# Attention and two MoE layers on one core: the first two token tiles of every expert done as one pair of 256 tokens

## The reference, cut to what matters

```python
noisy_logits = x @ w_gate + np.log1p(np.exp(x @ w_noise)) * noise
top2 = np.argpartition(-noisy_logits, 2, axis=1)[:, :2]      # weights: softmax over the two
for e in range(8):
    for k in range(2):
        mask = top2[:, k] == e
        h = np.maximum(x[mask] @ w1[e], 0.0)                 # 512 -> 1024
        out[mask] += top2_w[mask, k, None] * (h @ w2[e])     # 1024 -> 512
```

## Time and profile before

| | |
|---|---|
| time, median of 3 runs | 819.7 us (819.58 to 820.21) |
| the profiled execution's own time | 820.68 us |
| its span | 819.0 us |
| PE busy | 785.7 us (96%) |
| PEld busy | 624.8 us (76%) |
| DVE, ACT, POOL busy | 373.5, 333.2, 234.5 us |

### The profile page before, as it was taken

The page is one execution under the profiler, slowest core; times in us unless marked ns, Lnnn a source line. Parts: engine busy times, 40 slices in busy tenths (PEclk is TensorE's granted clock), DMA queues, the critical chain, the costliest instruction groups (busy, mean ns, idle before and its releaser), DMA issues.

```text
span 819.0 us, 11388 instructions
## 1 busy us (share of the span) xinstructions
PE 785.7 (96%) x4058; PEld 624.8 (76%) x4058; DVE 373.5 (46%) x674; ACT 333.2 (41%) x616; POOL 234.5 (29%) x428
## 2 busy tenths in 40 slices
PE   6999989999999999999999979999999999999993
PEld 4777657887788878888887768888888888888882
DVE  5777865542623225343254733545253354454221
ACT  4677864433251223431144532534343444443220
POOL 4478740000000300003202443334333343433331
PEclk9999999999999999999999999999999999999997
DMA  9878404410010000100135352546354364643120
GB/s 170 208 153 272 110 3 135 132 45 1 2 50 1 1 1 1 52 0 1 65 102 166 105 143 45 178 124 183 65 150 129 83 191 113 169 142 89 31 44 13
DMA packets 75874, 75.14 MB, mean 92 GB/s; under 512 B 45806, under 2 KB 53486, under 8 KB 75824
## 3 DMA queue, kind: packets, MB, share of 16 engines
q1 hardware_dynamic: 68416, 61.64, 25.5%
q0 software_dynamic: 7408, 12.88, 8.5%
HBM read 60.22 MB, written 14.28 MB: 91 GB/s over the span
## 4 chain that ended last, share of the span: by engine, by line
PE 83%; DVE 4%; SPq 3%; DMA 3%; issue 2%; ACT 2%; POOL 1%; POOLq 0%; ACTq 0%
PE banks L474 25%; PE banks L973 17%; PE banks L504 12%; PE banks L938 9%; PE banks L953 9%; PE banks L1427 2%; PE banks L1459 2%; PE banks L928 1%; PE banks L1439 1%; PE banks L967 1%; PE banks L949 1%; PE banks L522 1%; DMA rawv<-in_v_dram 1%; SPq L1270 1%; PE banks L1399 1%
## 5 line engine op out<-in xcount | busy, mean ns | idle before, releaser
L474 PE MATMUL banks<-XN,W_mid 128*128 128x512 f32 x552 | 135.3, 397 | 0.0
L973 PE MATMUL banks<-W_mid,XN 128*128 128x512 f32 x406 | 128.4, 405 | 0.0
L474 PEld LDWEIGHTS banks<-XN,W_mid 128*128 128x128 f32 x552 | 103.4, 188 | 25.7 <-issue 1.0
L365 POOL DMA_INDIRECT slots<-entry,slot_x x24 | 24.0, 1000 | 261.6 <-DVE slot_x L782 255.2
L1046 DVE TENSOR_TENSOR XN<-banks,XN 128x512 fp32r<-128x512 f32 x56 | 38.7, 691 | 118.7 <-ACT XN L1007 118.6
L973 PEld LDWEIGHTS banks<-W_mid,XN 128*128 128x128 f32 x406 | 74.4, 188 | 13.6
L1004 ACT ACTIVATE act_b<-banks 128x512 f32<-128x512 f32 x56 | 33.4, 597 | 109.8 <-PE banks L938 88.5
L973 PE MATMUL banks<-W,XN 128*128 128x512 f32 x240 | 77.2, 392 | 0.0
L474 PE MATMUL banks<-XN,W 128*128 128x512 f32 x288 | 73.6, 411 | 0.0
L474 PEld LDWEIGHTS banks<-XN,W 128*128 128x128 f32 x288 | 55.7, 196 | 13.5 <-issue 0.3
L599 ACT ACTIVATE HT<-act_b 128x512 fp32r<-128x512 f32 x36 | 22.8, 632 | 93.6 <-DVE act_b L703 93.6
(11 more groups left out here) (194 smaller groups left out, 1350.6 us busy)
## 6 DMA issues: line engine op xcount, KB each, us to landing
stage<-in_moe_w_dram SPq DMA_DIRECT2D x64, 512.0 KB
rawv<-in_v_dram SPq DMA_DIRECT2D x16, 192.0 KB, 3.9
out_dram<-zrow SPq DMA_DIRECT2D x1, 3072.0 KB, 12.3
moe_rows<-xT SPq DMA_DIRECT2D x12, 256.0 KB, 2.6
rawq<-in_q_dram SPq DMA_DIRECT2D x14, 192.0 KB, 3.6
rawk<-in_k_dram SPq DMA_DIRECT2D x14, 192.0 KB, 4.3
stage<-in_moe_w_gate_dram SPq DMA_DIRECT2D x4, 512.0 KB
stage<-in_moe_w_val_dram SPq DMA_DIRECT2D x4, 512.0 KB
```

What stands on the lines that cost most here:

```text
L474: last = nc.tensor.matmul(bank[2 * kind + n % 2][:], up_weight(kind, hw, k, c), xn[:, hx, k, :], start=(m == 0 and k == 0), stop=(m == 2 a ...
L973: last = nc.tensor.matmul(bank[5][:], he[:, hh, k, :], w2_part(e, hw, k), start=(q == 1), stop=(q == 24))
```

## The change

For each expert the first two tiles become one pair of 256 tokens. In the pair's first product the weights are stationary and the tokens move: for each of the 8 blocks of 128 hidden units 12 matmuls of 256 columns, two blocks to a PSUM bank. The result has the hidden units on the partitions, so it goes into the second product without transposes. The second product is that of two tiles, 24 matmuls of 512 columns each. What is left of an expert's tokens goes tile by tile as before (`one`). Two pairs, of expert 0 and of expert 1, now run before the routing of the third group is complete; the third tile of expert 1 comes next, then the rest of expert 0, then experts 2 to 7. The pair of expert e+1 has its rows gathered and turned during the pair of e. The w1 pieces of expert e+1 are split during the second product of pair e and the w2 pieces of e itself during its first product. The pairs have their own three row buffers and three result buffers; the tiles after them have one of each.

The core of the diff (new code, except the lines marked -):

```diff
+            def pair(e, between, before=None):                      # on PE
+                pe.wait_ge(sems["xbL"], 2 * e + 2)
+                pe.wait_ge(sems["wL"], NP1 - 6 + e * NP2 + NP2 // 2)
+                for fb in range(FC2):
+                    for m, (hw, hx) in enumerate(((0, 0), (1, 0), (0, 1))):
+                        for k in range(KC):
+                            last = nc.tensor.matmul(pair_bank(fb), expert_part(e, k, hw)[:, fb * P:(fb + 1) * P],
+                                                    xe_pair[:, hx, k, :], start=(m == 0 and k == 0),
+                                                    stop=(m == 2 and k == KC - 1))
+                    last.then_inc(sems["upT"], 1)
...
+                pe.wait_ge(sems["wL"], NP1 - 6 + (e + 1) * NP2)
...
+                for t in range(2):
+                    q = 0
+                    for k in range(FC2):
+                        if t == 0:
+                            pe.wait_ge(sems["hbL"], FC2 * e + k + 1)
+                        for m, (hh, hw) in enumerate(PASSES):
+                            if (t, q) in between:
+                                between[t, q]()
+                            q += 1
+                            last = nc.tensor.matmul(bank[5 + t][:], he_pair[:, k, hh, t * P:(t + 1) * P],
+                                                    w2_part(e, hw, k), start=(q == 1), stop=(q == 24))
...
+            pair(0, {(0, 8): row(2), (1, 8): row(3)})
+            pair(1, {(1, 8): first_ones, (1, 18): lambda: turn_one(1, rows_rest)})
+            n, before = tiles_of(pe, 1)
+            loop_one(1, n, before)
+            n, before = tiles_of(pe, 0)
+            one(0, before, 2, xe_rest, {2: row(4), 9: lambda: turn_one(before + 2), 16: row(5)}, 4)
+            loop_one(0, n, before)
+            for e in range(2, E):
+                n, before = tiles_of(pe, e)
+                between = {(1, 14): lambda: turn_one(before + e + 1)}
+                if e + 1 < E:
+                    between |= {(0, 8): row(2 * e + 2), (1, 4): row(2 * e + 3)}
+                pair(e, between, before)
+                loop_one(e, n, before)        # one(...) with turn_one(x) after its 10th L973-like matmul

+            def pair_hidden(e, fb):                                 # on ACT; its like on DVE waits for hbH
+                act.wait_ge(sems["upT"], FC2 * e + fb // 2 * 2 + 2)
+                nc.scalar.activation(he_pair[:, fb, 0], pair_bank(fb), ACT.Relu).then_inc(sems["hbH"], 1)
...
+                for fb in range(FC2):                               # ACT, pair e; DVE the same with _low
+                    pair_hidden(e, fb)
+                    if fb % 2 == 1:
+                        expert_high(act, e, 4 + fb // 2)
...
+                if e + 1 < E:                                       # DVE, after the hidden part of pair e
+                    pair_row_low(dve, 2 * e + 2)
+                    expert_low(dve, e + 1, 0)
+                pair_out(2 * e)
+                if e + 1 < E:
+                    expert_low(dve, e + 1, 1)
+                    pair_row_low(dve, 2 * e + 3)
+                    expert_low(dve, e + 1, 2)
+                one_row(before + e + 1)
+                if e + 1 < E:
+                    expert_low(dve, e + 1, 3)
+                pair_out(2 * e + 1)
+                loop_one(e, n, before)

-            def tile(J, entries, n, tokens=TOK):                    # on POOL
-                fetch(J, entries, n, tokens)
-                scatter(J)
-                shift(2)
...
+            def scatter_one(ap, s, c):
+                pool.wait_ge(sems["y1"], s + 2)
+                settle(c)
+                nc.gpsimd.indirect_dma_start(out, bass.IndirectOffsetOnAxis(ap=ap, axis=0), y_one, None,
...
+                                             compute_op=ALU.add).then_inc(sems["sc1"], 16)
+                pool.wait_ge(sems["sc1"], (s + 1) * 16)
+                settle(c + 1).then_inc(sems["free1"], 1)
+
+            def loop_one(e, n, before):
+                with pool.Fori(first_of_loop(e), n) as t:
...
+                    pool.wait_ge(sems["turn1"], one_turn(e, J))
...                                                                 # three copies: index, gate, next index
+                    settle(1)
+                    fetch_one(idx[:, 1:2])
+                    scatter_one(idx[:, 0:1], one_index(e, J), 2)
...
+            for i in range(4):
+                fetch_pair(i, GN * (NG - 1))
             send_entries(pool, NG - 1)
+            scatter_pair(0)
...
+                fetch_one(lst[:, e * NT + 2, 0:1])                  # POOL, experts 2 to 7
+                if e + 1 < E:
+                    fetch_pair(2 * e + 2)
+                    fetch_pair(2 * e + 3)
+                scatter_pair(2 * e)
+                scatter_pair(2 * e + 1)
+                loop_one(e, n, before)
```

More of the change, by code:

```diff
@@ L844, in dve_moe, with tiles_of @@
             dve_experts(dve, ranks, counts)
-        def expert_pieces(e, t):
-            return [(e + 1, j) for j in range(4 * t, 4 * t + 4)] if e + 1 < E and t < 2 else []
-        def tiles_of(eng, e, reads=True):
+        def tiles_of(eng, e):
+            eng.wait_ge(sems["cnt"], 1)
             n = eng.value_load(cnt_i[0:1, 0, e:e + 1])
-            first = eng.value_load(cnt_i[0:1, 1, e:e + 1])
-            return n, first
+            before = eng.value_load(cnt_i[0:1, 1, e:e + 1])
+            return n, before
@@ L856, in pool_experts, with first_of_loop @@
+        def first_of_loop(e):
+            return 3 if e == 0 else 2
         def pool_experts(pool):
-            pool.wait_ge(sems["ahead"], 16)
-            pool.wait_ge(sems["xm"], 16 * GT * (NG - 1))
[L859 to L896, removed]
@@ L989, in rows_high @@
[L989 to L1001 removed]
+                            last = nc.tensor.matmul(bank[5][:], he_one[:, hh, k, :], w2_part(e, hw, k),
+                                                    start=(q == 1), stop=(q == 24))
@@ new lines, in one, with loop_one, row, first_ones @@
+                last.then_inc(sems["l2e"], 1)
+            def loop_one(e, n, before):
+                with pe.Fori(first_of_loop(e), n) as t:
+                    J = before + t
+                    x = one_turn(e, J)
+                    one(e, one_index(e, J), x, xe_one, {10: lambda: turn_one(x)}, max(4, 2 * e + 2))
+            def row(i):
+                return lambda: turn_pair_row(pe, i)
+            def first_ones():
+                pe.wait_ge(sems["cnt"], 1)
+                turn_one(0)
@@ new lines, in act_experts @@
+            expert_high(act, 1, 3)
+            pair_row_high(act, 3)
+            for fb in range(FC2):
+                pair_hidden(1, fb)
+                if fb % 2 == 1:
+                    expert_high(act, 1, 4 + fb // 2)
+            one_row(0)
+            one_row(1, xe_rest)
+            n, before = tiles_of(act, 1)
+            loop_one(1, n, before)
+            n, before = tiles_of(act, 0)
+            one(before)
+            pair_row_high(act, 4)
+            expert_high(act, 2, 0)
```

453 lines of the change are left out of this document (285 added, 168 removed).

## The result

The changed kernel takes 893.07 us (median of 4 runs, 890.12 to 895.68), the kernel before 819.64 us; the ratio is 1.0874 (95% interval 1.0844 to 1.0904). It is slower by 73 us, where 892 was forecast. The profiled execution, the longest of the four, took 895.68 us, its span 893.8.

A forecast was written before the change was run, and what follows sets the result against it. PE was taken as the bound, busy 96% with no wait worth naming in a tile. Terms -5 + 26 + 43.7 - 9 + 17 = +72.7 on 819.7 gave 892 us; own range 870 to 915, widened to 855 to 920.

The forecast's parts named there:

- Step 1: PE's own work in a pair: 24.0 us against 24.66 for two tiles, a gain of 5 us over eight pairs.
- Step 2: Middle of a pair: PE waits 3.7 us for the last weight piece before the second product; seven pairs, 26 us.
- Step 3: Single tiles: PE waits for rows whose gather is issued only after the previous result's scatter landed; 43.7 us.
- 4, the start: Beginning of the experts: two pairs cover the routing; gain 9 us, at least 5, at most 11.
- Step 5: PE's clock: 19 new gaps of 2.6 to 4.3 us cost 0.9 us each in slow clock, 17 us; bounds 0 and 32.
- rival d: Pairs' first product: weight load and matmul take turns, 0.226 us each, 10 us more per pair; 972 us, chance 0.05.
- Rival c: Expert stage: weight pieces and POOL's chain do not bind PE; only fewer transposes and covered routing count; 806 us, chance 0.08.

The follow-up runs named there:

- e6_order: e3_both with ACT and DVE splitting the next single tile's rows and gating the pair's second result sooner; 821.04 us, ratio 0.9984 to the kernel before.
- e8_late: e6_order with the pair of expert 1 held back until the first routed single rows are gathered; 831.64 us, ratio 1.0129 to the kernel before.
- e4_fill: Changed kernel with matmuls on unused results ahead of the pairs' piece wait and the single tiles' row wait; 875.29 us, ratio 1.0619 to the kernel before.
- e2_pieces: Changed kernel with PE waiting for each w2 piece just before its first use, not for all eight; 875.75 us, ratio 1.0612 to the kernel before.
- e3_both: Changed kernel with the e2_pieces edit, and POOL waiting for a scatter's landing only after issuing the next gather; 829.54 us, ratio 1.0061 to the kernel before.

## Why the prediction was right

The direction, the two waits and the total were right. By its steps, with what the trace of the changed kernel and the experiments give:

| step | forecast, us | found, us |
|---|---|---|
| 1, PE's work in eight pairs | -5 | -6.5 (23.85 against 24.66 in e6_order; 341.0 against 347.5 in the table above) |
| 2, wait for the last piece | +26 | +25.6, seven waits |
| 3, rows of single tiles | +43.7 | +33.6, twelve waits |
| 4, the start | -9 | -8 to -9 (of the 11.3 lost before, 2.75 stay: the pair of expert 0 takes 26.75 us; e8_late: 10.6 for undoing it, 2.6 of slow clock included) |
| 5, clock | +17 | +27.4 behind the 19 gaps (windows); 24, with 3.3 left (e4_fill); 29 by what is left of the 73 |

**Step 1** took 0.122 us for a matmul of 256 columns with its own weight load. Measured are 96 in 11.5 us, 0.120. Load and matmul overlap, and rival d is out: 0.226 was its price. The Trainium skill ("TensorE: Matmul & The Clock Gate", "What overlaps and what doesn't") says that a weight load overlaps matmuls in flight only when it goes to other rows of the array. The traces disagree: each of these loads fills all 128 rows, and the matmuls follow at 0.120.

**Step 2** came out to a tenth: PE's first matmul 15.36 us after the pair's start (552.02 to 567.38), forecast 15.4. The forecast had ACT free and the piece landed both at 12.7; measured are 12.4 and 12.8, so the DMA came last by a little, and a shorter step from DVE to PE (0.24 instead of 0.33) made it up. e2_pieces shows it as a cause and not only as a place, but also that the 26 us do not come back alone: 18 of wait returned at the next places (10.5 for gathers, 5.8 for split rows, 2.0 for rows of the next pair).

**Step 3** had the chain right and one of its terms too large. The term is the gather: it took 2.2 and 2.8 us in the two tiles shown and 2.2 to 3.3 in all twelve, from its start to PE's turn, where I took 3.6, from between a loaded row and a lower bound of 2.55. The bound had no row behind it and was itself too high. The chain ahead of it was a little longer than I had it: 8.7 to the gather's start instead of 8.45 behind a single tile, 10.1 instead of 9.35 behind a pair, where the scatter starts late and takes 5.3 us. Together 10 us less: behind a single tile PE waited 1.8 to 2.7 us instead of 3.4, behind a pair of experts 2 to 6 3.2 to 4.2 instead of 4.3.

**Step 5** was too small by as much. I took 0.9 us for a gap, since I thought that part of a slow spell would fall in idle time. The windows of the changed kernel give 1.44 on average, and by place: each of the pairs' seven gaps of 3.5 to 4.0 us cost 1.7 to 1.8, 12.3 together. Of the twelve tiles seven lost 1.6 to 1.8, one 3.4 and four nothing, 15.1 together. The four had waited 1.8, 1.8, 1.9 and 2.7 us, and three of those that lost had waited only 1.9 to 2.1, so the length of the gap alone does not decide here. Steps 3 and 5 erred by 10 us each in opposite ways; that the total is 892 against 893 is luck, and the parts are right to 10 us.

**Rival c** was a version in which nothing waits and only steps 1 and 4 are left, 806 us. e3_both and e6_order come nearest to it and reach 829.5 and 821.0, so it was priced too low for what an edit of the order alone can reach: behind the two waits stood others of 8.5, 5.9 and 1.9 us. e6_order's two kinds of wait still hold 9.6 us (6.7 and 2.9) of its expert stage, which is 2.8 us shorter than that of the kernel before.

What stays open: why gaps of about 2 us cost clock in some tiles and not in others, and whether fillers of the right length would give back all of the 27 us and not only 21.

## What to carry to other kernels

Ask of every wait on a queue what is issued behind it: here a gather for the next tile stood behind the landing of the last result, and a whole product behind a weight piece that its last quarter uses. In a loop, work out the chain from the end of one round to the turn of the next in microseconds; the busy share of POOL, 23 to 29%, tells nothing of it. When PE is otherwise busy throughout, as here at 96%, most gaps also cost clock: the gaps of 3.1 us and more cost 1.6 to 3.4 us each, so one of 3 us is to be priced at 4.6 or more; and when one wait is taken away, look at once for the one that stood behind it.

## What the runs showed of the hardware

A gather of 128 rows of 2 KB was turned by PE 2.2 to 3.3 us after its DMA instruction started when no scatter was in flight (the changed kernel), 1.06 of it in the instruction; with a pair's scatter in flight it took 3.8 and 4.2 (e6_order). The scatter with add took 4.7 us at a DMA share of 0.42 (its own share included), 5.3 at 0.62 (the changed kernel) and 6.1 to 6.2 beside the transfers of weight pieces, at 0.77 and 0.91 (e6_order). Matmuls of 256 columns, each with a weight load of 128 rows, followed each other at 0.120 us (e3_both). Filling PE's gaps with matmuls on unused results, and nothing else, made the kernel 21 us faster: the granted clock rose from 0.955 to 0.982. The same program with the same waits had a granted clock of 0.955 on one chip and 0.946 on another, which cost 6 us.
